# Seventeen attention units ahead of the feed-forward steps instead of twenty, with the head's work put in another order on every engine

## The reference

```
for c in range(S // 32):                       # B=4, H=8, S=768, D=64
    k_full = concat(mem_k, k[c*32-16 : c*32+40]);  v_full likewise
    a = softmax(q_c @ k_full.T / sqrt(D));  out[c] = a @ v_full
x = out as [3072, 512]
h = x @ moe_w_in;  g = where(h > 0, h, exp(min(h, 0)) - 1);   x = g @ moe_w_out
h = x @ moe2_w_in; g = s * max(h, 0)**2 + b;                  out = g @ moe2_w_out
```

## Time and profile before

| | |
|---|---|
| time, median of 3 runs | 1222.36 us (1215.42 to 1224.62) |
| the profiled execution | 1217.71 us, span 1216.0 us |
| busy, share of the span | PE 92%, PEld 73%, DVE 70%, ACT 62%, POOL 35% |
| DMA | 302.80 MB, 249 GB/s over the span |
| granted TensorE clock, mean | 0.976 |

### The profile page before, as it was taken

The page is one execution under the profiler, slowest core; times in us unless marked ns, Lnnn a source line. Parts: engine busy times, 40 slices in busy tenths (PEclk is TensorE's granted clock), DMA queues, the critical chain, the costliest instruction groups (busy, mean ns, idle before and its releaser), DMA issues.

```text
span 1216.0 us, 18125 instructions
## 1 busy us (share of the span) xinstructions
PE 1124.5 (92%) x5809; PEld 884.5 (73%) x5809; DVE 854.7 (70%) x1246; ACT 753.6 (62%) x1767; POOL 425.1 (35%) x465
## 2 busy tenths in 40 slices
PE   7887779898999999989899998899999999999998
PEld 4655557676777778767688777677787887887876
DVE  4666628856996984996785975948948559567386
ACT  3675548666757866846756756636656466566463
POOL 5758627865124664625461064601002010000000
PEclk7998789998999999999999999999999999999999
DMA  9997679999889999978997589866577665686664
GB/s 215 275 238 182 207 234 334 307 347 301 260 226 314 327 299 302 339 241 303 346 284 236 173 265 387 266 190 182 180 218 269 192 191 175 198 232 191 191 190 156
DMA packets 203750, 302.80 MB, mean 249 GB/s; under 512 B 112520, under 2 KB 120712, under 8 KB 203656
## 3 DMA queue, kind: packets, MB, share of 16 engines
q1 hardware_dynamic: 203656, 301.65, 81.1%
HBM read 226.10 MB, written 75.50 MB: 248 GB/s over the span
## 4 chain that ended last, share of the span: by engine, by line
PE 66%; DVE 19%; DMA 6%; issue 5%; ACT 3%; POOL 1%; SPq 0%; ACTq 0%; DVEq 0%; POOLq 0%
PE ps L992 29%; PE ps L977 26%; DVE g_lo L1422 4%; DMA w_ring<-w_scratch 3%; PE ps L891 3%; DVE X L1334 2%; DVE att L1303 2%; DVE T L1417 2%; DVE X L1417 2%; PE ps L900 2%; PE ps L852 2%; PE ps L885 2%; DVE X L1391 1%; DVE xc_lo L1327 1%; DMA elu<-x_scratch 1%
## 5 line engine op out<-in xcount | busy, mean ns | idle before, releaser
L992 PE MATMUL ps<-g_hi,w_ring 128*128 128x512 f32 x1344 | 422.8, 396 | 29.7 <-issue 15.8
L977 PE MATMUL ps<-xc_hi,w_ring 128*128 128x512 f32 x1344 | 435.4, 397 | 15.6 <-DMA w_ring<-w_scratch 8.1
L992 PEld LDWEIGHTS ps<-g_hi,w_ring 128*128 128x128 f32 x1344 | 246.8, 188 | 97.1 <-issue 30.6
L977 PEld LDWEIGHTS ps<-xc_hi,w_ring 128*128 128x128 f32 x1344 | 254.2, 189 | 74.0 <-DMA w_ring<-w_scratch 11.0
L977 PE MATMUL ps<-xc_lo,w_ring 128*128 128x512 f32 x672 | 263.4, 392 | 0.0
L992 PE MATMUL ps<-g_lo,w_ring 128*128 128x512 f32 x672 | 262.4, 391 | 0.0
L1422 DVE TENSOR_TENSOR g_lo<-X,g_hi 128x512 fp32r<-128x512 f32 x240 | 185.0, 776 | 41.7 <-ACT g_hi L1187 40.9
L764 POOL TENSOR_TENSOR w_new<-w_raw,w_new 128x256 fp32r<-128x256 f32 x173 | 155.3, 902 | 156.2 <-ACT w_new L1200 152.0
L1187 ACT ACTIVATE g_hi<-X 128x512 fp32r<-128x512 f32 x240 | 149.5, 628 | 78.4 <-PE ps L992 75.8
L1334 DVE TENSOR_TENSOR X<-s,ps 128x512 f32<-128x512 f32 x144 | 96.0, 680 | 114.0 <-ACT s L1129 90.9
L992 PEld LDWEIGHTS ps<-g_lo,w_ring 128*128 128x128 f32 x672 | 126.3, 188 | 27.2
(11 more groups left out here) (114 smaller groups left out, 1417.6 us busy)
## 6 DMA issues: line engine op xcount, KB each, us to landing
w_ring<-w_scratch SPq DMA_DIRECT2D x336, 512.0 KB, 4.3
w_scratch<-w_new SPq DMA_DIRECT2D x173, 256.0 KB, 4.9
w_scratch<-att SPq DMA_DIRECT2D x51, 256.0 KB, 4.9
w_raw<-in_moe_w_in SPq DMA_DIRECT2D x16, 512.0 KB, 5.9
w_raw<-in_moe_w_out SPq DMA_DIRECT2D x16, 512.0 KB, 5.7
x_scratch<-y SPq DMA_DIRECT2D x3, 2048.0 KB, 10.0
att<-x_scratch SPq DMA_DIRECT2D x6, 1024.0 KB, 8.5
out<-elu SPq DMA_DIRECT2D x24, 256.0 KB, 4.4
```

Of the source, the lines that this page charges most:

```text
L977: last = nc.tensor.matmul(bank_of(st.pi, st.i), w[:, a, cols], x[:, st.pi, kk, :], start=(st.pi in (P1, P5, P4) and kk == 0 and n == 0), s ...
L992: last = nc.tensor.matmul(bank_of(st.pi, d), w[:, a, cols], x[:, k % RING, :], start=(st.pi in (P1, P5, P4) and st.i == 0 and n == 0), sto ...
```

## The change

It sets `HEAD` to 17 and weaves 15 units 12 steps apart instead of 12 units 14 apart. It gives each engine's head loop another order: PE puts the scores first, transposes probabilities two units behind and multiplies with v three units behind, with two idle products a unit instead of three; ACT copies and places before the splits and exponentials of the turn; DVE normalises after the next unit's maximum. `HEAD_SPLITS` has other turns, ACT places the last unit at step 3 and not before the steps, and ACT touches the table of exponentials first. POOL prepares five sets before both `sums_of_head`, not four before the first and one between. The head prepares 42 products instead of 49 and saves 39 of them ahead of the steps instead of 46. The waits that stood at product `HEAD_PREP` of `cut_w` move to the first products that need them. `hi_slot` has other slopes: the remaining 70 products of layer one follow every 1.1 steps instead of 63 every 1.2, with three more steps ahead of the last set, and layer two's are spread to step 405 instead of 376. `SPLIT_AT` of the first half moves from steps 90 to 99 to steps 92 to 100, and POOL's sums of tiles 2 to 4 move between other sets.

More of the change, by code:

```diff
@@ L184, in sets_of, with order_of @@
     return (PAIR, PAIR + 1) if m in (PAIR, PAIR + 1) else (m,)
-PREP = [(m, pi) for m0 in range(2 * SETS) if m0 == sets_of(m0)[0] for pi in PREPARED for m in sets_of(m0)]
+def order_of(ms):
+    return [(m, pi) for m in ms for pi in PREPARED[:2]] + [(m, pi) for pi in PREPARED[2:] for m in ms]
+PREP = [what for m in range(2 * SETS) if m == sets_of(m)[0] for what in order_of(sets_of(m))]
 PREP_AT = {what: pp for pp, what in enumerate(PREP)}
@@ L649, in load_x @@
                 else:
-                    wait_x0_saved(sp, UNITS - 1)
+                    if t == TPL:
+                        wait_x0_saved(sp, UNITS - 1)
+                        for pp in range(WIDE_END - SAVES - 3, WIDE_END):
+                            wait_w_saved(sp, pp)
                     sp.wait_ge(y_saved, 16 * (i + 1))
@@ L833, in _ @@
                 sums_of_x(1, kk)
-            for m in range(SETS, SETS + 8):
+            for m in range(SETS, SETS + 4):
                 prepare((m,))
@@ L837, in _ @@
                 sums_of_x(2, kk)
-            for m in range(SETS + 8, SETS + 12):
+            for m in range(SETS + 4, SETS + 8):
                 prepare((m,))
@@ L841, in _ @@
                 sums_of_x(3, kk)
-            for m in range(SETS + 12, 2 * SETS):
+            for m in range(SETS + 8, 2 * SETS - 2):
                 prepare((m,))
-            for t in range(4, TILES):
-                for kk in range(2):
-                    sums_of_x(t, kk)
+            sums_of_x(4, 0)
+            for m in range(2 * SETS - 2, 2 * SETS):
+                prepare((m,))
+            sums_of_x(4, 1)
+            for kk in range(2):
+                sums_of_x(5, kk)
         @block.tensor
@@ L1207, in copy_out @@
                 nc.scalar.activation(out_rows[n % 4], out_bank(t, tb)[:, :], ACT.Copy).then_inc(out_copied, 1)
+            act.wait_ge(ident_done, 1)
+            nc.scalar.activation(exp_table[:, :], zero[:, :], ACT.Exp)
             act.wait_ge(nat_zeros, 1)
-            for it in range(-2, HEAD + 3):
-                if it >= 3:
-                    place_x(it - 3)
+            for it in range(-1, HEAD + 3):
+                if 0 <= it - 3 < HEAD:
+                    copy_PT(it - 3)
+                if it >= 4:
+                    place_x(it - 4)
+                if 0 <= it + 1 < HEAD:
+                    copy_qT(it + 1)
+                for c, pi, at in HEAD_SPLITS:
+                    if at == it:
+                        split_head(c, pi)
                 if 0 <= it < HEAD:
@@ L1433, in _ @@
             dve.wait_ge(tiny_set, 1)
-            for it in range(-2, HEAD + 1):
-                if it >= 1:
-                    normalise(it - 1)
-                if it + 2 < HEAD:
-                    copy_kT(it + 2)
-                if 0 <= it + 1 < HEAD:
-                    maximum(it + 1)
-                if it >= 1:
-                    copy_PT(it - 1)
-                for c, pi, at in HEAD_SPLITS:
-                    if at == it:
-                        lo_head(c, pi)
+            for it in range(-1, HEAD + 4):
+                if 0 <= it + 1 < HEAD:
+                    copy_kT(it + 1)
+                if 0 <= it - 3 < HEAD:
+                    copy_PT(it - 3)
+                for c, pi, at in HEAD_SPLITS:
+                    if at == it - 1:
+                        lo_head(c, pi)
+                if 0 <= it < HEAD:
+                    maximum(it)
+                if 0 <= it - 1 < HEAD:
+                    normalise(it - 1)
             for g in range(STEPS + 2):
```

65 lines of the change are left out of this document (31 added, 34 removed).

## The result

The changed kernel takes 1213.04 us in the median (1208.42 to 1217.88), the kernel before 1220.29 beside it: ratio **0.995**, 95% interval 0.9927 to 0.9972. That is 0.5% faster where 2.3% were forecast (1193, range 1177 to 1211). The head came almost as forecast; it was given back in the weave.

The account below looks back on a forecast made before the run. Tile 0 was taken as bound by PE's order and what holds it up, the head's end by POOL, then SP. Terms -31.7+3.3-7.0-5.4-2.4+13.8+1.6+3 = -24.8 against 1217.7 gave 1193, range 1177 to 1211.

Parts of the forecast that it names:

- First matmul, -31.7 (116.4): End of the head: POOL's sets and sums, then SP's saves, put the first matmul at 116.4 us, not 148.12: -31.7.
- Half clock at the start +3.3, step 8 -7.0: PE begins step 0 at half clock after waiting: +3.3 us; ACT's step 8 wait for stored x goes: -7.0.
- Raw weights -5.4: Steps 56 to 69: ACT's wait for set 15's raw weights goes, -5.4 us, at worst -2.
- x -2.4: Split of tile 1's x comes two steps later; PE's wait behind it goes: -2.4 us, at worst 0.
- Three units +13.8: Weave: three more units among the steps at 4.6 us each, +13.8.
- The step that failed: Weave, units twelve steps apart: one normalisation more in the first down block, +1.6 us; waits of Q's and k's transposes, 0.
- DMA +3: Tile 0's denser transfers, at 352 GB/s, cost 0.5 us a unit, +3 in all.
- the starved ring: Rival: woven units in steps 14 to 82 cut tile 0's DMAs to 270 GB/s, 40 us in all: 1230, chance 0.05.
- The rival with full DMAs: Rival: tile 0 gets only 317 to 321 GB/s, units cost 16 us in all, not 3: 1208, chance 0.18.
- Layer two 0, between -3 and +3: Layer two's weight splits, spread anew, cost 0 us, between -3 and +3 by where they stand.
- The head at half clock: Rival: PE's clock falls to half in the head, step 0 comes at 132 us: 1205, chance 0.07.
- POOL runs freer: Rival: in the head POOL's sets end 8 to 10 us earlier, attention sets step 0: 1183, chance 0.17.

Follow-up runs that it names:

- ring_early: The change, with 35 saves of weights, not 39, ahead of the ring's loads in SyncE's list: 1205.9 us, ratio 0.9909.
- head_alone: The change's head order with before's 20 head units, 12 woven 14 steps apart, 49 products prepared, before's layer-two spread: 1208.9 us, ratio 0.9921.
- head19: sums_saves with one unit moved from the head into the weave (19 in the head, 13 woven): 1197.8 us, ratio 0.9833.
- apart12: head20_ring_early with its 12 woven units 12 steps apart, not 14: 1205.3 us, ratio 0.9904.
- head20_ring_early: head_alone with only 35 saves of weights ahead of the ring's loads in SyncE's list, not 42 to 46: 1191.8 us, ratio 0.978.
- layer2_before: The change, with layer two's preparations spread as in the kernel before and GpSimd's sums for x in before's order: 1213.6 us, ratio 0.9949.
- shift4: head20_ring_early with every woven unit 4 steps later, still 14 apart: 1195.5 us, ratio 0.9794.
- sums_saves: head20_ring_early with GpSimd's first four sums ahead of set 4 and only 32 saves, not 35, let ahead: 1194.9 us, ratio 0.981.

## Why the prediction was wrong, point by point

- **First matmul, -31.7 (116.4).** Right in its chain, 119.95 measured, 28.2 earlier. Set 4 took 15.7 us (79.9 to 95.6), not 12.9, the eight sums 11.3, not 10.1; the load landed sooner than 5.6. POOL's sums back to back, SP's pause moved away from 84 and PE's 9.8 us for the ring are as named, and ring_early shows the chain by cutting it. The attention's own end was not at 106 as argued: ScalarE had a second wait behind the same saves (10.9 us).
- **Half clock at the start +3.3, step 8 -7.0.** With the head these make -35.4 by step 13; measured -33.9. No wait for stored x at step 8 is left. The prediction's check "near 143" did not follow from that sum, which gives 148.4; 149.85 came.
- **Raw weights -5.4.** Right: in head_alone, with units where before had them, steps 56 to 69 took 23.5 us against 29.9.
- **x -2.4.** Its bound came, 0: steps 84 to 97 took 25.2 us against 27.8, but steps 98 to 111 26.8 against 24.2, so that the 28 steps took 52.0 in both. VectorE is busy 48.0 of these 52 us before and after.
- **Three units +13.8.** Not contradicted: the remainder is 13.0, one unit in head19 5.6.
- **The step that failed: "Twelve steps apart, the first down block ... gets one normalisation more, 1.6 ...: +1.6. Q's transposes now wait for the placing of the unit before, k's only for a copy; both come before they are needed, 0, as far as ACT is not late."** It priced the move of the old units to other steps at 1.6 us; twelve units 12 apart cost 16.3 more than 14 apart, and the denser weights, which it counted only as DMA load, 3.0. In tile 0 apart12 is 16.5 longer than head20_ring_early with about one unit more (989 groups on PE against 939), from step 112 to 195 as long (139.4 and 139.6) with about one unit less: at 4.6 a unit some 12 of the loss lie in tile 0, the rest in tile 1. So tile 1's 9.3 in the change, near the forecast, is in part luck. ScalarE is late, by 4 us at the split of w shown above, though it is busy only 133 of 196 us. The mean price of a unit, 4.6, was read from blocks of the earlier trace rows, all of which lie at the places of 10 + 14c; a dear one was in the same rows, 208.4:236.3, 27.9 us against 23.7, and was put down to VectorE's load. A price by place was to be read there.
- **DMA +3.** Not seen: PE has no wait for `w_ring` in steps 14 to 195, so the starved ring falls too. The rival with full DMAs gives a time near the measured one (1208), not its cause: the waits are for ScalarE and VectorE.
- **Layer two 0, between -3 and +3.** Tiles 2 and 3 lost 4.4, of which layer2_before gives back 1.6, but single executions with before's spread lie at 332.2 to 340.1 there: neither can be told from nothing, and the net of undoing the spread is nothing.
- **The head at half clock.** In part. The clock stays at its upper level while the turns run steadily, but the 0.89 from 40 to 84 is a stretch at the lower one, 74.65 to 84.89: PE had waited 2.25 us for a unit's memory keys until 75.21, and the turn from 77.73 then took 7.8 us, not 4.6. The chain through POOL covered it. The steady turns from 20 to 40 us:

```profile
20.00:40.00 20.00, 18.16 (x198) 13.35 (x196) 16.37 (x26) 17.13 (x84) 10.71 (x16) 1.00 1.09 246
```

The Trainium skill, "TensorE: Matmul & The Clock Gate", Part 4 (PE-mode transpose), says that a transpose doesn't count as busy in the same way as other matmuls and that the full clock doesn't engage for it. This row, at 1.00 with one idle product less a turn, doesn't show a loss by that, but it is no test of it either: of a turn's 52 matmuls 16 are transposes, 36 are not.
- **POOL runs freer.** No: set 3 ended at 79.9, set 4 later than priced.

As a balance of the profiled executions: 33.9 won by step 13; then lost 16.3 to the other steps of the units, 3.0 to density and 13.0 in the remainder put down to three units, won 5.2 by the old waits and 3.1 by which the change's execution is shorter than that of ring_early, from which the shares are taken (2.2 of it in steps 112 to 195, where the two have the same lists, so not explained): 24.0 lost; 0.9 won in steps 196 to 223, 4.4 lost in tiles 2 and 3; 6.5 are left. The median ratio, 0.995, is 6.1 us.

## What to carry to other kernels

A piece of work woven into a periodic list has no one price: read its price at each place of the period, and when the spacing is changed, price the pieces that only move. A shift by a few steps, with nothing else changed, is the cheapest experiment for that, if it is read wait by wait: shift4's price was one wait of another kind. Where an in-order queue waits for a slow producer, look at what stands behind it that does not need that producer: here one condition in SyncE's list was worth 17 us with twenty units in the head.

## What was not expected of the hardware

- A PE wait costs more than itself. Around the 2.63 us one the clock of ten us is 0.83, and in apart12 against head20_ring_early 11.4 us of idling brought 4.9 us of slower running:

```profile
212.00:222.00 10.00, 7.37 (x32) 5.09 (x28) 4.46 (x6) 4.84 (x11) 7.34 (x9) 0.83 0.95 333
```

- SyncE's issues themselves fill the head's end: in sums_saves 33 of them between 88.1 and 111.8 us take 19.5 us of its list, from 0.31 to 2.15 each. The last load of v there and the ring load behind it:

```profile
106.86 2.15 SPq L595 DMA_DIRECT2D X<-in_mem_v  x1
109.11 0.35 SPq L636 DMA_DIRECT2D w_ring<-w_scratch  x1
```
